# The first four attention steps of a fused attention and two-MLP kernel, rebuilt: loads, PSUM banks, mask order and sum of squares

## What is computed

```python
# q, k, v: (4, 8, 576, 64); window = 64
scores = scale * np.matmul(q, k.transpose(0, 1, 3, 2))
mask = (rel >= 0) & (rel < window)
attn = softmax(np.where(mask, scores, -1e9))       # with + 1e-9 in the denominator
x = (attn @ v) with the heads side by side          # (2304, 512)
xn = x / np.sqrt(np.mean(x * x, -1) + 1e-6) * rms_g
x = (silu(xn @ w_gate) * (xn @ w_val)) @ w_out      # 512 -> 1536 -> 512
h = x @ w_in
out = (h * sigmoid(1.702 * h)) @ w_out2             # 512 -> 2048 -> 512
```

## Time and profile before

| | |
|---|---|
| median of three runs | 980.57 us |
| profiled execution | 981.89 us |
| its span | 980.1 us |
| TensorE busy | 946.6 us (97%) |
| DVE, ScalarE, POOL busy | 406.0, 357.9, 109.1 us |
| mean granted TensorE clock | 0.98 of full |
| first gate matmul of the first MLP | 46.22 us from the span's start |
| DMA | 57.56 MB, mean 59 GB/s |

### The profile page before, as it was taken

The page is one execution under the profiler, slowest core; times in us unless marked ns, Lnnn a source line. Parts: engine busy times, 40 slices in busy tenths (PEclk is TensorE's granted clock), DMA queues, the critical chain, the costliest instruction groups (busy, mean ns, idle before and its releaser), DMA issues.

```text
span 980.1 us, 12296 instructions
## 1 busy us (share of the span) xinstructions
PE 946.6 (97%) x4750; PEld 798.3 (81%) x4750; DVE 406.0 (41%) x735; ACT 357.9 (37%) x747; POOL 109.1 (11%) x159
## 2 busy tenths in 40 slices
PE   4589999999999999999999999999999999999998
PEld 3489888888888888888888888888888888888897
DVE  1479754444444444443434454224223322422332
ACT  2266655444545345553411122223222222321232
POOL 4446400110010100101012220000000000000000
PEclk7599999999999999999999999999999999999999
DMA  4466311210222102210122323002000100100010
GB/s 134 133 193 202 122 57 57 68 58 11 78 68 70 44 11 89 70 44 11 43 93 82 114 78 108 1 1 87 1 1 35 51 1 1 65 1 1 0 44 22
DMA packets 33420, 57.56 MB, mean 59 GB/s; under 512 B 3409, under 2 KB 9041, under 8 KB 33361
## 3 DMA queue, kind: packets, MB, share of 16 engines
q1 hardware_dynamic: 33360, 56.77, 18.1%
HBM read 47.32 MB, written 9.44 MB: 58 GB/s over the span
## 4 chain that ended last, share of the span: by engine, by line
PE 91%; DVE 3%; issue 3%; POOL 2%; ACT 1%; POOLq 0%; DVEq 0%
PE ps L437 21%; PE ps L439 21%; PE ps L438 21%; PE ps L536 7%; PE ps L535 7%; PE ps L537 7%; PE ps L427 3%; PE ps L404 3%; PE ps L417 1%; DVE w_all L725 1%; PE ps L400 1%; ACT prob L556 1%; PE ps L434 1%; POOL sq L353 0%; DVE nmax L679 0%
## 5 line engine op out<-in xcount | busy, mean ns | idle before, releaser
L437 PE MATMUL ps<-x_hi,w_all 128*128 128x512 f32 (+1 forms) x800 | 301.7, 377 | 4.2 <-DVE x_lo L715 3.7
L439 PE MATMUL ps<-x_lo,w_all 128*128 128x512 f32 (+1 forms) x800 | 295.8, 370 | 0.0
L438 PE MATMUL ps<-x_hi,w_all 128*128 128x512 f32 (+1 forms) x800 | 295.3, 369 | 0.0
L437 PEld LDWEIGHTS ps<-x_hi,w_all 128*128 128x128 f32 x800 | 152.0, 190 | 29.1 <-issue 4.4
L439 PEld LDWEIGHTS ps<-x_lo,w_all 128*128 128x128 f32 x800 | 151.6, 189 | 25.9
L438 PEld LDWEIGHTS ps<-x_hi,w_all 128*128 128x128 f32 x800 | 152.0, 190 | 24.2
L812 DVE TENSOR_TENSOR hid<-ps,sig 128x512 f32<-128x512 f32 (+1 forms) x80 | 51.1, 638 | 208.0 <-ACT sig L642 207.8
L642 ACT ACTIVATE sig<-ps 128x512 f32<-128x512 f32 (+1 forms) x80 | 44.5, 556 | 215.8 <-PE ps L439 215.8
L535 PE MATMUL ps<-w_all,h_hi 128*128 128x512 f32 x288 | 112.2, 390 | 0.0
L536 PE MATMUL ps<-w_all,h_hi 128*128 128x512 f32 x288 | 112.2, 390 | 0.0
L537 PE MATMUL ps<-w_all,h_lo 128*128 128x512 f32 x288 | 112.0, 389 | 0.0
(11 more groups left out here) (71 smaller groups left out, 999.5 us busy)
## 6 DMA issues: line engine op xcount, KB each, us to landing
qbd<-in_q_bd SPq DMA_DIRECT2D x36, 256.0 KB, 2.7
wstage<-in_w_a SPq DMA_DIRECT2D x36, 256.0 KB, 3.2
vwin<-in_v_win SPq DMA_DIRECT2D x36, 256.0 KB, 2.7
wstage<-in_w_b SPq DMA_DIRECT2D x32, 256.0 KB, 3.0
kwin<-in_k_t SPq DMA_DIRECT2D x36, 160.0 KB, 2.8
out_dram<-late SPq DMA_DIRECT2D x18, 256.0 KB, 2.7
xT<-x_scratch SPq DMA_DIRECT2D x4, 1024.0 KB, 5.8
x_scratch<-wstage SPq DMA_DIRECT2D x3, 1024.0 KB, 4.2
```

The source lines that it names most:

```text
L437: pe.matmul(out_, w[:, 0, cols], xh, start=first, stop=False)
L438: pe.matmul(out_, w[:, 1, cols], xh, start=False, stop=False)
L439: return pe.matmul(out_, w[:, 0, cols], xl, start=False, stop=last)
```

## The change

All of it lies in the first four steps, but for names and the place of the mask matmul.

- Loads: q of steps 0, 1, 2 is issued on SP at once, k of 0, 1, 2 and v of 0, 1, 2 on ScalarE's queue, its table load between v 0 and v 1. Each has a semaphore of its own. Step 2's q, k, v lie in the second half of the weights' stage (`away`), so chunk 1 of the weights waits for `pv_done` 3. Step 3 takes step 0's q and k buffers after `scores_done` 1 and its v buffer after `pv_done` 1. Weight pieces (0, 0) and (0, 1) are issued behind `scores_done` 1, (0, 2) behind `pv_done` 1, and chunk 2 behind v of steps 4 and 5.
- Banks: scores 0 to 3 in banks 0 to 3, transposes in 4 and 5, outputs in 6 and 7. `prob` of steps 2 and 3 lies in unused columns of `xT`, and `probT` of steps 1 and 2 in `sig` and `hid`.
- TensorE runs all four scores first, then for each step transposes, products with v, and the sum of squares of the step before.
- Mask: q and k first, then one matmul of `both` (two 64-row identities side by side) with `mask`, whose upper 64 partitions are zero. DVE zeroes the tiles and copies the masks, POOL makes six selects ahead of `ident`.
- Squares: each early step has a tile of squares of its own, and four matmuls with `ones` add up in bank 0. POOL's adds are gone from the early steps.
- Evacuations: both halves of the early outputs go to ScalarE, after all four `exponentials`. POOL's first weight copies come after `normalise(3)`. DVE's order is written out anew; `weights_lo_A(0, 2)` comes after `split_x_lo(0)`. The sigmoid table is loaded after `split_x_hi(0)`.

```diff
         def s_bank(s):
-            return 0 if s < EARLY and s % 2 else S_BANK
+            return s if s < EARLY else S_BANK
         def pt_bank(s):
-            return 1 if s < EARLY and s % 2 else PO_BANK
+            return 4 + s % 2 if s < EARLY else PO_BANK
         def o_bank(s):
-            return 2 + s % 2 if s < EARLY else PO_BANK
+            return 6 + s % 2 if s < EARLY else PO_BANK
+        AWAY = 2
+        away = wstage[:, 3 * DM:6 * DM]
+        def ring(s):
+            return 0 if s == EARLY - 1 else s % 2
+        def load_k_early(eng, s):
+            group, c = divmod(s, PAIRS)
+            eng.dma_start(k_of(s), k_t[c, :, group * GT:group * GT + GT + BLK]).then_inc(k_early_loaded[s], 16)
             def load_wA(c, m):
                 if c >= 2:
                     sp.wait_ge(w_split, splitsA(c - 2, m))
+                elif c == 1:
+                    sp.wait_ge(pv_done, AWAY + 1)
...
-            load_qk(0)
+            for s in range(AWAY + 1):
+                load_q_early(s)
+            sp.dma_start(gcol[:, :], rms_g).then_inc(g_loaded, 16)
+            sp.wait_ge(scores_done, 1)
+            load_q_early(EARLY - 1)
+            load_k_early(sp, EARLY - 1)
             load_wA(0, 0)
-            load_v(0)
-            load_qk(1)
             load_wA(0, 1)
-            load_v(1)
-            sp.dma_start(gcol[:, :], rms_g).then_inc(g_loaded, 16)
-            for s in range(2, EARLY):
-                load_qk(s)
-                load_v(s)
-                load_wA(0, 2) if s == 2 else load_wA(1, 0)
-            load_wA(1, 1)
-            load_wA(1, 2)
+            sp.wait_ge(pv_done, 1)
+            load_v_early(sp, EARLY - 1)
+            load_wA(0, 2)
             load_qk(EARLY)
+            load_qk(EARLY + 1)
+            for m in range(3):
+                load_wA(1, m)
             load_v(EARLY)
-            load_qk(EARLY + 1)
             load_v(EARLY + 1)
-            load_wA(2, 0)
-            load_wA(2, 1)
-            load_wA(2, 2)
+            for m in range(3):
+                load_wA(2, m)
...
             normalise(0)
-            weights_hi_A(0)
-            for s in range(1, EARLY):
-                normalise(s)
-                squares(s - 1)
-            squares(EARLY - 1)
-            weights_hi_A(1)
-            weights_hi_A(2)
+            normalise(1)
+            squares(0)
+            normalise(2)
+            squares(1)
+            normalise(3)
+            weights_hi_A(0, 0)
+            squares(2)
+            weights_hi_A(0, 1)
+            squares(3)
+            weights_hi_A(0, 2)
+            for c in range(1, 3):
+                for m in range(3):
+                    weights_hi_A(c, m)
...
+                for i in range(GB):
+                    pe.matmul(bank[:, i, :], q_of(s)[:, i * P:(i + 1) * P], k_of(s)[:, i * BLK:i * BLK + P],
+                              start=(i == 0), stop=False, skip_group_check=True)
                 if s == 0:
-                    pe.wait_ge(consts_ready, 1)
+                    pe.wait_ge(both_ready, 1)
+                    pe.wait_ge(masks_copied, 1)
...
+                pe.matmul(bank, both[:, :], mask[:, from_:from_ + GB, :], start=False, stop=True,
+                          skip_group_check=True).then_inc(scores_done, 1)
...
+            def sum_squares_early(s):
+                pe.wait_ge(squares_done, s + 1)
+                ins = pe.matmul(ps[:, 0, 0:GT], ones[:, :], sq_of(s), start=(s == 0), stop=(s == EARLY - 1),
+                                skip_group_check=True)
+                if s == EARLY - 1:
+                    ins.then_inc(sumsq_done, 1)
...
+            for s in range(EARLY):
+                scores(s)
             pe.wait_ge(ident_ready, 1)
-            scores(0)
+            pe.wait_ge(consts_ready, 1)
             for s in range(EARLY):
-                if s + 1 < EARLY:
-                    scores(s + 1)
                 transpose_probs(s)
                 probs_by_v(s)
-            sum_squares(0)
+                if s >= 1:
+                    sum_squares_early(s - 1)
+            sum_squares_early(EARLY - 1)
...
+            for s in range(AWAY + 1):
+                load_k_early(act, s)
+            load_v_early(act, 0)
             nc.scalar.preload_act_table_set(EXP_SET)
-            for s in range(EARLY + 1):
-                if s < EARLY:
-                    exponentials(s)
-                if s >= 1:
-                    evacuate_o(act, nc.scalar.copy, 1, s - 1)
+            load_v_early(act, 1)
+            load_v_early(act, AWAY)
+            for s in range(EARLY):
+                exponentials(s)
+            for s in range(EARLY):
+                for h in range(2):
+                    evacuate_o(act, nc.scalar.copy, h, s)
             inverse_rms(0)
-            nc.scalar.preload_act_table_set(SIGMOID_SET)
             act.wait_ge(g_loaded, 16)
             split_x_hi(0, TILES_A[0][1], True)
+            nc.scalar.preload_act_table_set(SIGMOID_SET)
...
             row_max(0)
-            for s in range(EARLY):
-                if s + 1 < EARLY:
-                    row_max(s + 1)
-                reciprocal_of_sum(s)
-                if s >= 1:
-                    evacuate_o(dve, nc.vector.tensor_copy, 0, s - 1)
-                evacuate_probT(s)
-            evacuate_o(dve, nc.vector.tensor_copy, 0, EARLY - 1)
-            weights_lo_A(0)
+            row_max(1)
+            reciprocal_of_sum(0)
+            row_max(2)
+            evacuate_probT(0)
+            reciprocal_of_sum(1)
+            row_max(3)
+            evacuate_probT(1)
+            reciprocal_of_sum(2)
+            evacuate_probT(2)
+            reciprocal_of_sum(3)
+            evacuate_probT(3)
+            weights_lo_A(0, 0)
+            weights_lo_A(0, 1)
             scale_x(0)
             dve.wait_ge(g_loaded, 16)
             split_x_lo(0, TILES_A[0][1], True)
-            weights_lo_A(1)
+            weights_lo_A(0, 2)
+            for m in range(3):
+                weights_lo_A(1, m)
```

More of the change, by code:

```diff
@@ L300, in then @@
                 pool.wait_ge(pool_order, order[0])
-            then(nc.gpsimd.memset(ident[:, :], 0.0))
+            rows = slice(0, BLK)
+            pool.wait_ge(zeros_made, 1)
+            then(nc.gpsimd.affine_select(out=mask[rows, 2, :], in_=mask[rows, 2, :],
+                                         compare_op=ALU.is_ge, fill=NEG, base=BLK,
+                                         pattern=[[-1, P]], channel_multiplier=1))
+            nc.gpsimd.affine_select(out=mask[rows, 2, :], in_=mask[rows, 2, :],
+                                    compare_op=ALU.is_gt, fill=NEG, base=0,
+                                    pattern=[[1, P]], channel_multiplier=-1).then_inc(masks_made, 1)
@@ new lines, in _ @@
+            then(nc.gpsimd.affine_select(out=mask[rows, 3, :], in_=mask[rows, 3, :],
+                                         compare_op=ALU.is_ge, fill=NEG, base=BLK,
+                                         pattern=[[-1, P]], channel_multiplier=1))
+            then(nc.gpsimd.affine_select(out=mask[rows, 3, :], in_=mask[rows, 3, :],
+                                         compare_op=ALU.is_ge, fill=NEG, base=-BLK,
+                                         pattern=[[1, P]], channel_multiplier=0))
@@ L303, in _ @@
+            then(nc.gpsimd.affine_select(out=both[rows, :], in_=both[rows, :], compare_op=ALU.not_equal, fill=1.0,
+                                         base=0, pattern=[[-1, P]], channel_multiplier=1))
+            nc.gpsimd.affine_select(out=both[rows, :], in_=both[rows, :], compare_op=ALU.not_equal, fill=1.0,
+                                    base=BLK, pattern=[[-1, P]], channel_multiplier=1).then_inc(both_ready, 1)
             nc.gpsimd.affine_select(out=ident[:, :], in_=ident[:, :], compare_op=ALU.not_equal, fill=1.0,
@@ L304, in _ @@
                                     base=0, pattern=[[-1, P]], channel_multiplier=1).then_inc(ident_ready, 1)
[L305 to L319, removed]
@@ L355, in squares, with weights_hi_A @@
                 nc.gpsimd.tensor_tensor(part, part, sq[:, :], ALU.add).then_inc(squares_done, 1)
-            def weights_hi_A(c):
-                for m in range(3):
-                    pool.wait_ge(w_loaded[c % 2][m], 16 * (c // 2 + 1))
-                    nc.gpsimd.tensor_copy(slotA(c)[:, m, 0, :], raw(c % 2, m)).then_inc(w_hi_made, 1)
+            def weights_hi_A(c, m):
+                pool.wait_ge(w_loaded[c % 2][m], 16 * (c // 2 + 1))
+                nc.gpsimd.tensor_copy(slotA(c)[:, m, 0, :], raw(c % 2, m)).then_inc(w_hi_made, 1)
             def weights_hi_B(f):
@@ L720, in split_x_lo, with weights_lo_A @@
                                                 ALU.subtract).then_inc(x_lo_ready, 1)
[L722 to L726 removed]
+            def weights_lo_A(c, m):
+                dve.wait_ge(w_hi_made, splitsA(c, m))
+                nc.vector.tensor_tensor(slotA(c)[:, m, 1, :], raw(c % 2, m), slotA(c)[:, m, 0, :].bitcast(F32),
```

(27 more changed lines are left out.)

155 lines of the change are left out of this document (86 added, 69 removed).

## The result

The changed kernel takes 963.98 us, the median of four runs (963.38 to 965.37), beside 981.13 for the kernel before: ratio 0.9823, 95% interval 0.9808 to 0.9837. That is 17.1 us off. The forecast was 12 off, at 968.6; the range down to 962.5 holds the time, with 1.5 us to spare at its lower edge. The profiled execution took 963.56, its span is 961.8; that is 18.30 less than the span of the profiled execution before, which lay 0.8 above its median.

A forecast was written before the change was run, and what follows sets the result against it. TensorE bounds the body; the 46 us ahead of it are latency. L moving from 42.5 to 30.5 takes 12.0 off the profiled 981.89, giving 969.9, or 968.6 as timed median; range 962.5 to 974.5.

The forecast's parts named there:

- Body untouched, the shift of L is the change: TensorE-bound body: edits there cost nothing, so the 12.0 us gained by L arrive at the end.
- L: Start of ScalarE's Ln after the early steps: 42.52 us before, forecast 30.5, ends 26 and 33.3.
- Loads: Start of the kernel: q0 and k0 land at 4.0 us, third pair by about 7.5, before TensorE wants it.
- Masks under the load: POOL's six selects at the start end at 3.9 us, constants needed at about 5.7: no cost.
- The two long waits: Early steps: 6.25 us blamed on POOL's weight copies and queues, 6.42 us on reciprocals behind the next step's row maxima.
- Which rate?: TensorE's clock in the early steps: full for last scores, steps 0 and 1, half for most of the rest; L 30.5.
- the first rival: TensorE at the full rate through the early steps: L = 26, 16.5 us off, 964.1; chance 15%.
- one step of the softmax chain: Early steps 1 to 3, transposes, copy, products with v and a sum: 5.1 us each at half rate, 3.1 at full.
- The wait that the change adds: Early steps: the first transposes stand up to 1.8 us behind the scores of step 3.
- Four sums for three adds: Squares of the early steps: four TensorE sums of 1.24 us replace one, a loss of 3.7 at half rate.
- After L, nothing: From L into the first weight pass: table load, DVE's order and chunk 2's late third cost nothing, 2.3 us to spare.
- The rival of starving weights: Weight loads come late, 1.5 us lost on each of ten chunks, 983.6; chance 4%.

The follow-up runs named there:

- the filled kernels: Extra bf16 matmuls of a zeroed tile added in TensorE's idle stretches; the kernel before with them took 973.30 us, ratio 0.9921.

## Why the prediction came out as it did, step by step

- **Body untouched, the shift of L is the change: held in the main, with 2 us on top that the sum had at nothing.** 16.34 of the 18.30 are at L. Of the rest, 1.50 are in the first pass. The rate can account for part: before, the gate matmuls ran at the lower level until 50.84, 4.6 us, now until 33.13, 2.9 us, some 0.8 us of work. But the kernel before with POOL's order alone, which has the old body, took 82.46 there in place of 83.83, so the 1.50 may not be the change's at all. The last 0.79, from the first sigmoid of 512 to the end, was costed at nothing. It is 849.21 to 849.26 in all eleven traces with the new body, and 849.99 to 850.05 in all three with the old. In the rows, kernel before and then changed, from the matmul ahead of the scores to the second one behind them:

```profile
135.06 0.39 PE L439 MATMUL ps<-x_lo,w_all 128*128 128x512 f32 x1
135.29 0.39 PE L400 MATMUL ps<-mask,identb 128*128 128x512 bf16 x1
...
136.65 0.40 PE L438 MATMUL ps<-x_hi,w_all 128*128 128x512 f32 x1
```

```profile
117.55 0.39 PE L498 MATMUL ps<-x_lo,w_all 128*128 128x512 f32 x1
117.78 1.05 PE L447 MATMUL ps<-kwin,qbd 128*128 128x128 f32 x8
...
119.11 0.39 PE L497 MATMUL ps<-x_hi,w_all 128*128 128x512 f32 x1
```

  That is 1.59 and 1.56 us, so the mask last costs TensorE a little less. Over the 24 steps that lie there it adds up: from the matmul ahead of the scores of the first to that of the last are 309.98 us before (135.06 to 445.04) and 309.21 in the changed kernel (117.55 to 426.76), 0.77 or 0.03 a step, which is all but 0.02 of the 0.79. No run changed the mask's place alone, so that it is the mask is argued from the rows.
- **Loads: held.** k 0 landed at 4.25 (forecast 4.0), scores 0 started at 4.38, the third pair was there when wanted. `scores(3)` started at 10.37, forecast 10.2 to 10.6; in other traces of this order their k came as late as 11.11.
- **Masks under the load: held.** POOL's six selects ended at 3.78.
- **The two long waits: the first was misread.** Its cause is the order of scores, as for the second; the loop over the weights held `normalise(1)` for 0.8 us (1.8 with the clock held). The sum did not use the loop's price, so the number was not hurt.
- **"Which rate?": this step failed.** It chose the upper level for the last scores and steps 0 and 1 and the lower one for the rest, L = 30.5. The trace has the upper level from the third scores to L = 26.18, and the first rival, built from the same rows at the upper rate, said 26 and 964.1. Nearly all of the 4.3 us between forecast and L are this choice. The argument for the lower level was a break of 0.83 us in each step of 5.1; in this execution such breaks did not bring the clock down, in the second one it fell for some 3 us. The rule that speaks for the rival in the Trainium skill (TensorE: Matmul & The Clock Gate, What's actually happening), that activity releases a clock which is throttled by default, was weighed and given 15%; the trace agrees, with the rise in the third scores. That the rival's 964.1 is within 0.2 of the time is partly luck: it counts 16.5 off, where the spans differ by 18.30 and the medians by 17.1.
- **The term mis-sized is one step of the softmax chain**: the forecast took 5.1 us at the lower rate for steps 2 and 3 and 4.1 for step 1; the trace has 2.9 from T of step 2 to T of step 3 (18.31 and 21.24). Of the 3.1 forecast at the upper rate it is 0.2 less.
- **The wait that the change adds, and `squares(0)` before `normalise(2)`: held.** `normalise(0)` ended at 11.33 and the transposes began at 11.55, so of the wait of up to 1.8 only 0.2 came, as the scores were done at 11.7 (forecast 11.3 to 12 where the rate rises on the way). `normalise(2)` was forecast to end at 17.9 and ended at 18.25; taking that wait away moved L by 1.07.
- **Four sums for three adds, a loss of 3.7 at the lower rate: wrong in sign as the kernel runs.** With the clock at 1.00 the sums cost L 0.9 less than the adds. No run compares the two at the lower rate.
- **After L, nothing: held for the weights.** POOL had copied the last third of chunk 2 by 35.20, L + 9.0 (forecast L + 9.3), and DVE did not wait for it. The rival of starving weights did not come.

What stays open is the first pass. It took from 81.3 to 84.0 us over the fourteen traces, and two of the longest three, 83.81 and 84.03, belong to the two kernels with the earliest L (the third is the 83.83 of the kernel before). In the changed kernel DVE is busy for 8.5 to 9.4 of each 10 us from 50 to 90, and POOL's copies wait for loads in nearly every chunk. In all six kernels and executions whose gate starts ahead of 31 us the second pass opens between 111.19 and 112.95; that DVE or the loads set such a floor fits the numbers and was not tested.

## What to carry to other kernels

Ahead of a body that one engine bounds, look for the engine order that puts the independent first stage of a later step behind the last stage of an earlier one; here, scores first was worth 6 us with the clock held and 13 as it falls, against 4 and 3.4 for more buffers, loads, banks and the rest together. Price such a stretch at both clock levels and let the rows of an unbroken run decide, since packing it changes the rate as well as the waits. Before blaming a queue for a wait, check that the instruction said to be ready is of the same step: count the instances of its line.

## What the runs showed of the hardware

- The granted clock stayed at 1.00 from 10 to 28 us in one execution with TensorE busy for 1.91 of 3, 2.52 of 4 and 3.12 of 4 us in successive stretches, and was 0.59 on average in 20 to 24 in another execution of the same kernel, with 1.94 of 3 and 2.52 of 4 in the two stretches ahead. So such a stretch can run at either level.
- Matmuls of zeros went with the upper level: once it was reached, the granted clock stayed at 1.00 in each of the filled kernels, and in the kernel before they took 7.8 us off the time (0.9921) while adding work. The first twelve, from 1.19 us, took 5.30 us, 0.44 each; nine of them at 8.98 took 2.10, 0.23 each.
- POOL's square of 128 x 256 in the changed kernel's first pass took 2.20 us beside DVE's subtractions with two SBUF inputs (from 56.77), and 0.61 beside DVE's row maxima, which read PSUM (from 51.89). In the kernel before it was 2.20 and 0.61 as well.
